# Routing worked out tile by tile inside the token mix, with expert row lists, a row gather and an eight-chunk weight ring

## The reference

```python
# 1. local attention: chunks of 32 queries see 8 memory keys, 16 keys to the left, 8 to the right
a = softmax(scale * q_c @ k_full.T);  out[:, :, c] = a @ v_full
# 2. token mix
xk = mu_k * x + (1 - mu_k) * x_prev;  xr = mu_r * x + (1 - mu_r) * x_prev
x2 = sigmoid(xr @ w_r) * (relu(xk @ w_k) ** 2 @ w_v)
# 3. one of 8 experts per token, with a choice that can be carried over from the token before
for b in range(B):
    prev_e = -1
    for s in range(S):
        fresh_e = int(np.argmax(logits[b, s]))
        e = fresh_e if s == 0 or local_gate[b, s] < 0.5 else prev_e
        prev_e = e
        h = np.maximum(x[b, s] @ w1[e], 0.0)
        out[b, s] = p[e] * (h @ w2[e])
```

## Time and profile before

| what | value |
|---|---|
| median of 3 runs | 556.85 us |
| span of the profiled execution | 553.9 us |
| TensorE busy (matmul) | 446.1 us, 81% |
| VectorE, ScalarE, GpSimd busy | 247.3, 214.1, 50.8 us |
| mean granted TensorE clock | 0.910 of full speed |
| DMA | 67.26 MB, mean 121 GB/s |

### The profile page before, as it was taken

How to read it: one execution, slowest core, us unless ns; L and a number is a source line. 1 busy time by engine, 2 the same in 40 slices (tenths; PEclk the granted TensorE clock), 3 DMA queues, 4 the chain that set the end, 5 groups by cost and what they waited for, 6 DMA issues and landing times.

```text
span 553.9 us, 10631 instructions
## 1 busy us (share of the span) xinstructions
PE 446.1 (81%) x3759; PEld 368.3 (66%) x3760; DVE 247.3 (45%) x478; ACT 214.1 (39%) x320; POOL 50.8 (9%) x62
## 2 busy tenths in 40 slices
PE   1757639999999999999500589999899989898772
PEld 1645529798989989898300467777678767676552
DVE  2545576544425344431451455222642364646661
ACT  1333466635243343431111453223432345435640
POOL 0000000010101010100035001111111101111010
PEclk9887759999999999999755679999999999999987
DMA  8687533272000000000057845111551155554640
GB/s 316 220 284 245 199 122 112 72 279 103 0 0 0 0 0 0 0 1 2 0 159 229 292 161 197 63 47 30 185 194 38 38 190 179 188 178 148 217 161 10
DMA packets 18309, 67.26 MB, mean 121 GB/s; under 512 B 2734, under 2 KB 2734, under 8 KB 18288
## 3 DMA queue, kind: packets, MB, share of 16 engines
q1 hardware_dynamic: 13104, 50.92, 27.2%
q0 software_dynamic: 4896, 16.05, 8.5%
q10 hardware_dynamic: 288, 0.02, 0.0%
HBM read 55.41 MB, written 12.62 MB: 123 GB/s over the span
## 4 chain that ended last, share of the span: by engine, by line
PE 54%; DMA 17%; issue 9%; DVE 8%; ACT 4%; POOL 2%; DVEq 2%; ACTq 2%; SPq 1%; POOLq 0%
PE PS L407 12%; PE PS L534 10%; PE PS L439 10%; PE PS L517 7%; DMA QK<-tiles 5%; PE PS L423 5%; DMA XR<-grouped_rows 4%; DMA ERAW<-wexp 3%; DVE ELO L1036 2%; POOL grouped_rows L1131 2%; DMA rows_out<-OSB,OIDX 2%; PE PS L525 2%; PE PS L457 2%; ACT EHI L701 2%; PE PS L334 1%
## 5 line engine op out<-in xcount | busy, mean ns | idle before, releaser
L1036 DVE TENSOR_TENSOR ELO<-ERAW,EHI 128x1024 f32 (+1 forms) x56 | 66.6, 1222 | 40.3 <-ACT EHI L701 23.0
L701 ACT ACTIVATE EHI<-ERAW 128x1024 f32 (+1 forms) x56 | 56.8, 1052 | 42.6 <-DMA ERAW<-wexp 31.4
L517 PE MATMUL PS<-EHI,XSH 128*128 128x512 f32 x128 | 55.1, 430 | 7.7 <-DVE XSL L1044 7.7
L534 PE MATMUL PS<-EHI,HH 128*128 128x512 f32 x128 | 54.8, 428 | 5.6 <-DVE ELO L1036 4.9
L407 PE MATMUL PS<-XHI,WHI 128*128 128x256 f32 x192 | 56.5, 294 | 1.2 <-DVE WLO L819 1.2
L1057 DVE TENSOR_TENSOR HL<-PS,HH 128x512 fp32r<-128x512 f32 x32 | 22.1, 690 | 76.3 <-ACT HH L721 76.3
L407 PE MATMUL PS<-XLO,WHI 128*128 128x256 f32 x192 | 55.1, 287 | 0.0
L407 PE MATMUL PS<-XHI,WLO 128*128 128x256 f32 x192 | 55.1, 287 | 0.0
L517 PE MATMUL PS<-ELO,XSH 128*128 128x512 f32 x128 | 52.6, 411 | 0.0
L517 PE MATMUL PS<-EHI,XSL 128*128 128x512 f32 x128 | 52.6, 411 | 0.0
L534 PE MATMUL PS<-ELO,HH 128*128 128x512 f32 x128 | 50.6, 395 | 0.0
(11 more groups left out here) (144 smaller groups left out, 760.4 us busy)
## 6 DMA issues: line engine op xcount, KB each, us to landing
ERAW<-wexp SPq DMA_DIRECT2D x56, 512.0 KB, 4.4
QK<-tiles SPq DMA_DIRECT2D x12, 768.0 KB, 5.7
VV<-tiles SPq DMA_DIRECT2D x12, 520.0 KB, 3.7
grouped_rows<-ZR POOLq DMA_DIRECT2D x1, 5140.0 KB, 18.3
RAW<-wmix SPq DMA_DIRECT2D x10, 512.0 KB, 3.8
XR<-grouped_rows POOLq DMA_DIRECT2D x17, 257.0 KB, 3.1
CO<-consts SPq DMA_DIRECT2D x1, 470.0 KB, 5.3
rows_out<-OSB,OIDX POOLq DMA_INDIRECT x16, 2.8
```

The lines of the kernel that those rows point to most:

```text
L517: last = nc.tensor.matmul(PS[part][:, :], x[:, k, :], ww[:, c:c + 512], start=n == 0, stop=n == 11)
L534: last = nc.tensor.matmul(PS[4][:, :], x[:, f, :], ww[:, c:c + D], start=n == 0, stop=n == 23)
L701: nc.scalar.activation(EHI[w][:, ds(j * CH2, CH2)], ERAW[i][:], ACT.Copy).then_inc(ehi_done, 1)
L1036: nc.vector.tensor_tensor(ELO[w][:, ds(j * CH2, CH2)], ERAW[i][:], EHI[w][:, ds(j * CH2, CH2)].bitcast(F32), ALU.subtract).then_inc(elo_do ...
```

## The change

Four things are done.

1. **Routing moves into the mix.** The logits of a tile are used at once. `flags`, `state`, `one_hot`, `probs` and `place_rows` on VectorE and `flags_turned`, `state_turned` and `ranked` on TensorE work on one tile each, in between the next pair's work. A running sum of one-hots over tiles (SUM) gives each token its rank within its expert. The mix loops are unrolled. `down` now writes the PSUM banks that `gate` used, so `gate(g, u)` waits for x2 of the pair before and `down(g, u)` for the sigmoid.
2. **A fixed list region per expert.** A DRAM tensor `expert_lists` has 1536 rows of 16 words for each expert. For each token only 16 words (probability, token number) are scattered, tile by tile. The region is filled with an out-of-range number at the start.
3. **Rows are gathered through the list.** SP stores X2F to DRAM tile by tile. For each slot GpSimd loads 128 list rows (METL), makes integer row numbers (XIDX) and gathers the rows with an indirect DMA. The output scatter of a slot is issued after the gather of the next, and its landing is waited for by VectorE alone.
4. **Eight raw weight buffers.** NRAW goes from 4 to 8. All eight chunks of the first expert are issued at once, and the next expert's chunks are all split in the last slot of the current one.

TensorE, mix:

```diff
+            def ranked(t):
+                pe.wait_ge(onehot_done, t + 1)
+                if t % 2 == 0:
+                    pe.wait_ge(onehot_done, t + 2)
+                if t:
+                    pe.wait_ge(rows_ready, t)
+                nc.tensor.matmul(PS[7][:, 8:8 + NE], ones, SUM[:, t, :], start=True, stop=False)
+                nc.tensor.matmul(PS[7][:, 8:8 + NE], CO[:, C_LT:C_LT + P], OH[:, t, :], start=False,
+                                 stop=True).then_inc(rank_out, 1)
...
                 up(g, 1, first)
                 if not first:
-                    logits(2 * g - 1, 1)
+                    logits(b)
+                    flags_turned(a)
                 up(g, 2, first)
+                if not first:
+                    flags_turned(b)
                 up(g, 3, first)
-                for u in range(2):
-                    gate(g, u, first)
-                for u in range(2):
-                    down(g, u, first)
...
+                if not first:
+                    state_turned(a)
+                gate(g, 0, first)
+                if not first:
+                    state_turned(b)
+                gate(g, 1, first)
+                if not first:
+                    ranked(a)
+                down(g, 0, first)
+                if not first:
+                    ranked(b)
+                if last:
+                    down(g, 1, first, range(0, 9))
+                    x2_transposed(2 * g)
+                    down(g, 1, first, range(9, 18))
+                    logits(2 * g)
+                    down(g, 1, first, range(18, 24))
                 else:
...
+                    down(g, 1, first)
+                    x2_transposed(2 * g)
+            over_unrolled(mix)
+            flags_turned(NT - 2)
+            x2_transposed(NT - 1)
+            state_turned(NT - 2)
+            logits(NT - 1)
+            flags_turned(NT - 1)
+            state_turned(NT - 1)
+            ranked(NT - 2)
+            ranked(NT - 1)
+            nc.tensor.matmul(PS[6][:, 0:NE], ones, SUM[:, NT, :], start=True, stop=True).then_inc(count_out, 1)
```

VectorE, mix (a and b are the two tiles of the pair before):

```diff
                 squared(g, 0, first)
                 if not first:
-                    logits_out(2 * g - 2)
+                    flags(a)
...
                 squared(g, 1, first)
                 if not first:
-                    logits_out(2 * g - 1)
+                    state(a)
+                    flags(b)
...
+                else:
+                    state(b)
+                    one_hot(a)
+                    probs(a)
                 if not last:
                     mix_full(g + 1, 0, False)
+                if not first:
+                    one_hot(b)
+                    probs(b)
+                    place_rows(a)
+                if not last:
                     mix_full(g + 1, 1, False)
                     mix_lo(g + 1, 0, False)
                 gated(g, 0, first)
+                if not first:
+                    place_rows(b)
```

GpSimd (lists blanked at the start, list rows scattered as tiles come, then per slot):

```diff
+            for t in range(NT):
+                pool.wait_ge(rows_ready, t + 1)
+                pool.indirect_dma_start(MD, bass.IndirectOffsetOnAxis(ap=POSI[:, t:t + 1], axis=0),
+                                        MT[:, t, :], None).then_inc(rows_scattered, 16)
             pool.wait_ge(rows_scattered, 16 * NT)
...
+            with pool.Fori(0, NE) as e:
+                n = pool.value_load(RT[0:1, ds(e, 1)], min_val=0, max_val=NT)
+                first = pool.value_load(RT[0:1, ds(e + NE, 1)], min_val=0, max_val=NSLOT)
+                x = pool.value_load(RT[0:1, ds(e + 2 * NE + 1, 1)], min_val=0, max_val=NE - 1)
+                with pool.If(n > 0):
+                    with pool.Fori(0, n) as k:
+                        s = first + k
+                        pool.wait_ge(meta_done, s + 1)
+                        pool.dma_start(METL[:], MD[ds(x * CAP + k * P, P), :]).then_inc(metl_loaded, 16)
+                        pool.wait_ge(metl_loaded, 16 * s + 16)
...
+                        nc.gpsimd.tensor_copy(XIDX[:], METL[:, 1:2]).then_inc(xidx_done, 1)
+                        pool.wait_ge(xidx_done, s + 1)
...
+                        pool.indirect_dma_start(XR[:], None, XD,
+                                                bass.IndirectOffsetOnAxis(ap=XIDX[:, 0:1], axis=0),
+                                                bounds_check=last_row, oob_is_err=False).then_inc(xr_loaded, 16)
+                        scatter_out(s)
```

SP, ScalarE and VectorE around the weights:

```diff
-NRAW = 4
+NRAW = 8
...
+            for t in range(NT):
+                sp.wait_ge(x2_done, t + 1)
+                sp.dma_start(XD[t * P:(t + 1) * P, :], X2F[t % 2][:]).then_inc(x2_stored[t % 2], 16)
...
             for c in range(N2):
-                if c == NRAW:
-                    sp.wait_ge(xr_loaded, 16)
...
+                def next_lo(k, chunks):
+                    with dve.If(following > 0):
+                        with dve.If(k > n - 2):
+                            for i in chunks:
+                                expert_lo(e + 1, i, 1 - w)
```

More of the change, by code:

```diff
@@ L83, in moe_program @@
         CO = place("CO", [P, CW])
-        X2R = place("X2R", [P, NT, XGW])
         LG = place("LG", [P, NT, NE + 1])
@@ L123, in moe_program @@
         SG = [place(f"SG{i}", [P, D]) for i in range(2)]
-        X2F = [place(f"X2F{i}", [P, D]) for i in range(2)]
         X2T = [place(f"X2T{i}", [P, KT, P]) for i in range(2)]
@@ L130, in moe_program @@
         ERAW = [place(f"ERAW{i}", [P, CH2]) for i in range(NRAW)]
-        XR = place("XR", [P, XGW])
         XSH = place("XSH", [P, KT, P], F32R)
@@ L138, in moe_program @@
         OIDX = place("OIDX", [P, 1], I32)
[L140 to L145 removed]
+        XD = nc.dram_tensor("x2_rows", [B * S, D], F32, kind="Internal").ap()
+        MD = nc.dram_tensor("expert_lists", [NE * CAP, ROW], F32, kind="Internal").ap()
         PS = [pb(f"PS{i}") for i in range(8)]
@@ L183, in moe_program @@
         x2_done = sem("x2_done")
-        x2r_done = sem("x2r_done")
+        x2_stored = [sem(f"x2_stored{i}") for i in range(2)]
         x2t_done = sem("x2t_done")
@@ L213, in moe_program, with over_unrolled @@
         scattered = sem("scattered")
-        osb_free = sem("osb_free")
+        def over_unrolled(body):
+            for g in range(NPAIR):
+                body(g, g == 0, g == NPAIR - 1)
         def over_pairs(eng, body):
@@ L676, in mix @@
                     relu_square(g, q, first)
+                    if q == 2 and not first:
+                        route_exps(a)
+                        route_exps(b)
                 if first:
@@ L932, in te @@
-            def te(v):
-                return v.rearrange("p (t e) -> p t e", e=NE)
+            over_unrolled(mix)
+            state(NT - 2)
+            one_hot(NT - 2)
+            probs(NT - 2)
+            flags(NT - 1)
+            state(NT - 1)
+            one_hot(NT - 1)
+            place_rows(NT - 2)
+            probs(NT - 1)
+            place_rows(NT - 1)
             def et(v):
                 return v.rearrange("p (e t) -> p e t", e=NE)
-            def along(v, n):
-                return v.rearrange("p (t o) -> p t o", o=1).to_broadcast([P, v.shape[1], n])
@@ L1069, in _, with expert @@
             total = dve.value_load(RT[0:1, 2 * NE:2 * NE + 1], min_val=NT, max_val=NSLOT)
-            def expert(e, w, split):
+            def expert(e, w, more):
                 n, first = slots_of(dve, e)
-                if split:
-                    following = total - first - n
-                def split_next(turn, part):
-                    for i in (2 * part, 2 * part + 1):
-                        expert_lo(e + 1, NRAW * turn + i, i, 1 - w)
+                following = total - first - n
+                def next_lo(k, chunks):
+                    with dve.If(following > 0):
+                        with dve.If(k > n - 2):
+                            for i in chunks:
+                                expert_lo(e + 1, i, 1 - w)
                 with dve.If(n > 0):
```

498 lines of the change are left out of this document (245 added, 253 removed).

## The result

The changed kernel takes 630.03 us (median of 4 runs, 628.08 to 633.27). The kernel before, on the same chip, takes 556.23 (554.69 to 557.2). The ratio is 1.135, interval 1.130 to 1.140: 73.8 us slower. I had forecast slower, but by 31 us, and the time lies 22 us above the top of my range. The profiled execution has a span of 629.7 against 553.9 us and a mean granted clock of 0.882 against 0.910.

What follows compares the result with a forecast made beforehand. TensorE was taken to bound the mix and undisturbed slots. Terms 1.5 + 10.5 + 19 + 5 - 15.1 - 6.6 + 17 = +31.3, with 553.9 and 3.0, gave 588 us; 8-in-10 range 560 to 608.

Steps and rivals of the forecast that it cites:

- the tail: Last mix product to the first slot's first product: 27.6 us against 44.0, counted as -15.1 us (-20 to -11).
- the clock behind the stalls of `ranked`: Mix, pairs 1 to 4: TensorE at half clock after three of four idle stretches, 1.7 us each, +5 us (0 to 8).
- the routing products: Mix, five pairs: small transposes and products in TensorE's queue, 1.7 us plus late waits, 2.1 a pair, +10.5 us.
- The stalls of `ranked`: Mix, pairs 1 to 4: TensorE idles 4.7 us before `ranked(a)`, waiting for VectorE's one-hots behind `mix_full`; +19 us.
- what stays covered: Mix: X2F stores, list scatters of the first eleven tiles and ScalarE's exponentials hide behind other work; 0 us.
- The first slot: First slot, to its last product: 15.5 us against 22, weights arriving earlier but clock still cold; -6.6 us (-8 to -3).
- The fifteen slots: Slots after the first: 213 us becomes 230, through waits for rows, mostly at expert changes; +17 us (-8 to +30).
- the ring: GpSimd's slot loop of output scatter, list load, conversion and gather: 13.4 us in quiet slots, 17 in an expert's last slot.
- the ring binds everywhere: Rival, slots: list load and gather take 4.3 us each, every slot 15 to 17; 614 us, chance 0.11.
- it does not bind: Rival, slots: list load and gather are quick, fifteen slots take 209 us, -4 instead of +17; 567 us, chance 0.14.
- The rival on the faster side: Slots at TensorE's 12.8 us, clock kept in the mix, small products hidden; 543.5 us, chance 0.10.
- The start: Before the mix: blanking the lists, 0.79 MB, delays the query loads; +1.5 us (0 to 3).

Runs made afterwards that it cites:

- the filler: Changed kernel with 18 unread products of 128 x 512 put ahead of `ranked(a)` in pairs 1 to 4; 615.14 us, ratio 1.107.
- the six edits: Changed kernel with one-hots first, sigmoids between splits, later scatter, chunks 4 to 7 held for rows, blanking in the mix, low parts reordered; 542.01 us, ratio 0.974.
- the three edits: Changed kernel with both tiles' one-hots ahead of `mix_full`, sigmoids between weight splits and output scatter one slot later; 549.59 us, ratio 0.988.

## Why the prediction was right or wrong

The span grew by 75.8 us, and the prediction had 31.3. The 44.5 us between them lie in the slots (18.8), the tail (7.4), the first pair (6.1), the clock behind the stalls of `ranked` (5.8), the routing products (5.1) and, under 2 us together, the rest. One step failed in more places than any other: the price of the half clock behind a wait of TensorE. The prediction had 5 us for it in the mix and three times 1.7 in the slots; the runs show 10.8 and 18.

**The stalls of `ranked`, right.** The mechanism, the four pairs and the size stand: 18.8 us against 19.

**The clock behind them, mis-sized.** I took three of four stalls at 1.7 us. The clock fell behind all four, and each cost 2.7, as the filler shows: 10.8 against 5. I had half clock last 3.5 us; it lasted some 5.6 us behind the restart. The step that failed was reading as a lottery: a stall of 2.99 us had kept the clock there, and I let that stand for one in four here. The rows for a 4.49 us stall showed half clock, and these stalls are 4.5 long. The price was read from a single window, not from a stretch; `down` took 7.90 instead of 5.55.

**The routing products, mis-sized.** 3.1 us a pair against 2.1, over five pairs 5 us more. The late flags were 0.32 and 0.24 by the trace against my 0.4 in all, so the products, transposes and their hand-overs are 2.5 against 1.7. I had taken queued small transposes at 0.17, below the only row that I had, 0.23.

**The first pair, a missing step.** The prediction prices nothing there. The wait of the first `down` for a sigmoid was visible in the code and ScalarE's order in that pair had three weight splits in front. It cost 6.1 us against the kernel before, and the edit that removes it shortens the pair by 6.7. Under "what stays covered" I priced an exponential in front of a relu, but I did not go through each new wait of TensorE to ask what stands ahead of its releaser.

**The tail, right in order, mis-sized in the loads.** The table came 14.1 us after the last mix product (13.1 forecast). The list load took 6.50 against my 3.5, and the gather 6.86 against 4.4. These two terms are 5.5 of the 7.4 us missed; the rest is the later table, 1.0, and a list load that was issued 3.5 after the table instead of 2.6. My upper row for a load under weight traffic, 4.26, came from a stretch with four chunks on their way; with eight it was no bound.

By the Trainium skill, DMA: Bandwidth & Descriptors, section on the anatomy of a SWDGE transfer, with about 2.0 us plus bytes over 436e9 per DMA, an estimate for the list load is 2.0 us and for the gather 2.6. In the quiet slot below the list's 2.15 agrees and the gather's 3.42 does not; under weight traffic, 6.50 and 6.86 here, neither does.

**The first slot, right.** 16.0 us, a gain of 6.5 against 6.6.

**The fifteen slots, right in the ring, wrong in the clock behind its stalls.** A quiet slot and the transition of the first expert, each from one OSB to the next, in the chain of the changed kernel. They answer to the earlier trace rows.

```profile
383.65 0.75 DVE OSB L1156
...
386.29 2.15 DMA METL<-expert_lists
...
389.61 3.42 DMA XR<-x_rows,XIDX
...
393.73 2.75 PE PS L586 x12
```

```profile
409.24 0.75 DVE OSB L1156
...
414.20 3.67 DMA METL<-expert_lists
...
419.04 4.23 DMA XR<-x_rows,XIDX
...
423.31 1.12 PE PS L560 x4
424.42 5.08 PE PS L586 x12
429.63 0.75 DVE OSB L1156
```

The five quiet slots average 13.0 us against 13.4. At the transition, 14.07 us pass from OSB to the transposes of the rows, and the forecast has 17 - 3.4 = 13.6. So every part of the ring was sized well (issue, list, conversion, gather). But the transposes and the twelve y products then take 1.12 and 5.08 instead of 0.66 and 2.75, at a granted clock of 0.52: 6.3 us to the next OSB, not 3.4. The six last slots average 19.9 us against 17.1, which is 16.5 of the missing 19.

The slots behind the transitions take 17.5 against 15, another 7. The next chain piece there has both again: a list load of 3.71 us while the weights of the next expert are on their way (281 GB/s in that window), and 4.36 for the twelve products. Quiet slots and the last one give 2.7 back. In the sum I had also rounded 228 + 5 down to 230.

The term for the clock here was three stalls at 1.7. The trace has eight waits for rows of 2.3 to 4.5 us in the slots, and the experiment with the later scatter gave back 18 us of busy time beyond them. By cause and not by slot, that is some 13 of the 18.8 us missed here.

The prediction also held that the eight buffers remove the waits for weights. Two remained, 3.3 us each, in one-slot experts, where TensorE waits for low parts that VectorE has not yet made. In the first of them the rows come later still (a further wait of 2.3), so the ring sets that slot's length. In the next one no wait for rows of over a microsecond is left. It takes 18.9 us, and 17.6 in the kernel with the later scatter, where the same wait of 3.2 stands: here the low part sets most of the excess, which the prediction had at nothing.

**The rivals.** That the ring binds everywhere, with slots of 15 to 17 us, did not hold: the quiet slots take 13.0, 0.4 us more than in the kernel with the later scatter. Its 614 lies nearest to what was measured, but by another way. That it does not bind did not hold in this kernel, but its price is that of the kernel with the scatter one slot later: 202 us for the slots, where that rival had 209. The rival on the faster side gave 543.5, and the six edits take 542.0, but that the two meet is luck. The rival kept the 19 us of stalls, which the edits remove, and wanted slots of 195 where they have 199.6 and the small products hidden where each pair still stands 3.1 us above 30.46. Its condition, 5.9 us for list load, conversion and gather even at transitions, also left out the 2 us of register loads there. What the six edits do show is that the change can be made faster than the kernel before by the order of its work.

**The start** cost 2.4 against 1.5, from the blanking beside the query loads; moving it brought back 2 to 3 us, as said above.

## What to carry to other kernels

When work is moved into the queue of the engine that sets the time, write down for each new wait what stands ahead of its releaser on the releaser's own engine; two such places cost 36 us here, by the stretches that shrank when each was mended (29.6 and 6.7), and both went away by changing the order of a few lines. Price every idle stretch of TensorE together with the work behind it at half clock, which here added more than half again to the wait (2.7 to 4.7 us in the mix, 18 to 28.8 in the slots). And in a loop that loads for the next turn and stores for this one, put the load that others depend on ahead of the store that waits: that was worth 45 us here. More weight buffers brought nothing in the kernel before and some 13 us with the three edits, this one among them.

## What the runs showed of the hardware

- A stall of TensorE of 4.46 us in a stretch of full work was followed by some 5.6 us of work at a granted clock of 0.50, and 24 products took 7.90 instead of 5.55 us. With filler products in the same place the clock stayed at 1.00.
- In the fifteen slots the same 900 products kept TensorE busy for 209.9 us with eight waits of 2.3 to 4.5 us for rows between them, and for 191.8 us without these waits.
- A load of 8 KB by GpSimd took 2.15 us in a quiet slot, behind one output scatter, 3.67 beside the next expert's weights and 6.50 beside the first expert's eight chunks. When the chunks were held back until it was done, it took 1.87.
- A gather of 128 rows took 3.42 us in a quiet slot, 3.97 beside four chunks and 6.86 beside the eight chunks.
- From the start of OSB to the list load it took 2.6 us in a quiet slot (383.65 to 386.29) and 5.0 where three registers are read from the table (409.24 to 414.20).
- Six kernels with the same code in the fifteen slots (the changed one and five experiments) had slot sums from 243.6 to 251.6 us; a difference of a few us there proves nothing.
